# Attention taken two heads at a time, scores on halves of the array rows, values stationary, rows masked and exponentiated in place

## The chip, the cores and the metric

One Trainium2 chip, one of its cores. The metric is device time in microseconds (us) of one execution of the whole program, median of the runs shown.

## What is computed

Three stages follow one another. The first is attention in which each query keeps the keys of its 32 largest scores:

```python
# q, k, v: (2, 8, 576, 64)
scores = scale * np.matmul(q, k.transpose(0, 1, 3, 2))
kth = np.partition(scores, -top_k, axis=-1)[..., -top_k:-top_k + 1]
scores = np.where(scores >= kth, scores, -1000000000.0)
attn = np.exp(scores - np.max(scores, axis=-1, keepdims=True))
attn = attn / (np.sum(attn, axis=-1, keepdims=True) + 1e-09)
attn_out = np.matmul(attn, v)
```

The second takes the 1152 rows of 512 values, divides each by its root mean square, and passes it through a gated layer with 1536 hidden values: `silu(xn @ w_gate) * (xn @ w_val) @ w_out`. The third sends each row to one of 8 experts (the largest of 8 router logits), to at most 288 rows each, applies two matrices with a relu between them, and scales the row by its router probability.

## The kernel before

Rows are worked in nine tiles of 128. Tile 4 is the mixed one: its first 64 rows belong to batch 0 and its last 64 to batch 1, and the TensorE operations that depend on the batch are done for each half on 64 columns of the array (`halves`).

Attention and the gated layer run together in one list of steps, one head a step, 72 heads in all. In step n TensorE scores head n (`scores`, 128 rows of stationary queries, the other head's 64 rows of `q_cols` being zeros), ScalarE copies the scores into a ring of four rows `s_ring`, VectorE finds the 32nd largest in pairs of heads (MAX8 and MATCH_REPLACE8 in turn, then a last MAX8 that releases `th_set`), and ScalarE exponentiates into `p_ring` (L794). GpSimd turns the scores into ones and zeros by comparing with the threshold (L1120) and multiplies the exponentials by them (L1122). Four steps after the scores TensorE transposes the masked row in five blocks (`turn_probs`, L416), ScalarE copies them into `pt_ring`, and TensorE multiplies them as stationary operand with the values and a column of ones (`values`, L424, 65 columns). The ones give the sum of the row, and VectorE divides by it for a whole tile at a time (L966).

`due(n, offset)` says which tile's piece of the gated layer belongs to step n. A tile has six `ffn_block`s (gate and value columns 0 to 2, each twelve one-pass products of 512 columns: high part with high and low weights, L441 and L442, and low part with high weights, L445), 12 products for the output (`ffn_out`, L452), transposes of four blocks through the one bank `tb` (`turn`, L387; queries, normed rows, three of hidden values, output), router logits (L519), and the ranks. `use` numbers the turns of `tb`; each user waits on `t_free` for the one before.

In the first steps the two gated weights are scaled and split into a high and a low part, in twelve pieces. ScalarE writes the high part (L811); for six pieces it also scales the raw weights and GpSimd subtracts (L1113), for the six of `VEC_PIECES` VectorE does both in one operation (L912). The gated layer of the first tile waits for them.

After the last tile is dispatched the expert loop runs; the change leaves it as it is.

## Time and profile before

| | |
|---|---|
| median of 3 runs | 726.35 us (724.54 to 726.97) |
| profiled execution: its own time | 726.65 us |
| its span, first to last instruction | 724.9 us |
| mean granted TensorE clock | 0.956 of full speed |
| busy: TensorE / VectorE / ScalarE / GpSimd | 661.2 / 479.6 / 266.0 / 284.1 us |

Busy time is counted from the start of an instruction to its modelled end; matmuls are pipelined, so their shown durations overlap, and the distance between two starts is what one costs in a full queue. A granted clock of 1.00 is 2.4 GHz, 0.50 is 1.2 GHz. A number of instructions stands behind an x.

### The profile page before, as it was taken

The page shows a single profiled execution, that of the slowest core. Times are in us where ns is not written, and L with a number is a line of the kernel's source. Part 1 is how long each engine was busy: PE and PEld are TensorE (multiplying, and loading weights), DVE is VectorE, ACT ScalarE, POOL GpSimd, SP SyncE. Part 2 cuts the span into 40 slices and gives each one's busy share as a digit, 9 for nine tenths or more (in the row PEclk, how much of TensorE's full clock was granted, in tenths as well). Part 3 has the DMA queues.
Part 4 walks back from the last instruction along what each step waited for, and adds up shares of the span by engine and source line. Part 5 has one row for each costly group of instructions (what it writes and reads, how often), then busy time and mean ns, then how long its engine had stood idle before and what let it go on. Part 6 is the DMA issues. An engine that isn't in the chain of part 4 may idle for free.

```text
span 724.9 us, 10575 instructions
## 1 busy us (share of the span) xinstructions
PE 661.2 (91%) x3862; PEld 542.7 (75%) x3862; DVE 479.6 (66%) x1092; ACT 266.0 (37%) x473; POOL 284.1 (39%) x234
## 2 busy tenths in 40 slices
PE   5495689999999999999999999999985999999994
PEld 3374567688687578688688687785745999999994
DVE  3999979989989979989989999872211011111110
ACT  4385466355354354354354354432210011111110
POOL 2566765554645545546455564650000011111001
PEclk9878689999999999999999999999995999999998
DMA  9999000000000000000000000000067577876501
GB/s 186 364 382 291 0 16 0 1 16 1 7 23 1 16 16 1 16 16 1 15 16 1 16 2 1 15 1 16 0 247 236 195 247 262 270 251 232 185 16 35
DMA packets 52908, 65.43 MB, mean 90 GB/s; under 512 B 32058, under 2 KB 32058, under 8 KB 52860
## 3 DMA queue, kind: packets, MB, share of 16 engines
q1 hardware_dynamic: 51116, 60.05, 26.1%
q0 software_dynamic: 1744, 4.76, 1.8%
q8 instruction: 28, 0.46, 0.3%
q14 instruction: 20, 0.16, 0.1%
HBM read 52.89 MB, written 12.30 MB: 90 GB/s over the span
## 4 chain that ended last, share of the span: by engine, by line
PE 80%; DVE 13%; ACT 2%; DMA 1%; issue 1%; POOL 1%; SPq 0%; POOLq 0%; DVEq 0%; ACTq 0%
PE ps L452 13%; PE ps L595 10%; PE ps L609 10%; PE ps L424 8%; PE ps L400 8%; PE ps L441 6%; PE ps L445 6%; PE ps L442 6%; PE ps L416 5%; PE ps L387 3%; DVE w_top L1009 3%; DVE m L1004 3%; DVE w_parts L912 3%; DVE w_top L996 2%; DVE m L985 1%
## 5 line engine op out<-in xcount | busy, mean ns | idle before, releaser
L1120 POOL TENSOR_SCALAR s_ring<-s_ring,m 128x576 f32<-128x576 f32 x72 | 126.2, 1753 | 167.7 <-DVE m L1013 149.3
L1009 DVE MATCH_REPLACE8 w_top<-m,w_top 128x576 f32<-128x576 f32 x144 | 105.8, 743 | 0.0
L1122 POOL TENSOR_TENSOR p_ring<-p_ring,s_ring 128x576 f32<-128x576 f32 x72 | 102.3, 1420 | 6.0
L424 PEld LDWEIGHTS ps<-arena,pt_ring 128*128 128x128 f32 (+1 forms) x800 | 90.5, 186 | 16.8 <-issue 9.1
L1004 DVE MAX8 m<-w_top 128x8 f32<-128x576 f32 x144 | 101.6, 747 | 0.0
L424 PE MATMUL ps<-arena,pt_ring 128*128 128x65 f32 (+1 forms) x800 | 92.0, 267 | 4.1 <-ACT pt_ring L668 4.1
L452 PE MATMUL ps<-wo_space,hid 128*128 128x512 f32 x216 | 95.7, 593 | 0.0
L400 PE MATMUL ps<-arena,q_cols 128*128 128x288 f32 (+1 forms) x320 | 91.7, 442 | 2.1 <-ACT q_cols L668 1.4
L441 PE MATMUL ps<-w_parts,x_hi 128*128 128x512 f32 x216 | 92.2, 427 | 1.2 <-ACT x_hi L668 0.8
L442 PE MATMUL ps<-w_parts,x_hi 128*128 128x512 f32 x216 | 85.1, 394 | 0.0
L668 ACT ACTIVATE pt_ring<-ps 128x640 f32<-128x640 f32 x72 | 50.6, 703 | 81.0 <-PE ps L416 80.8
L595 PE MATMUL ps<-arena,w_loads 128*128 128x168 f32 x512 | 76.6, 312 | 0.6 <-ACT arena L668 0.6
L1129 POOL DMA_INDIRECT out_rows<-arena,s_ring x16 | 15.1, 942 | 157.9 <-DVE arena L1032 155.5
L609 PE MATMUL ps<-arena,w_loads 128*128 128x168 f32 x512 | 75.8, 307 | 0.6 <-issue 0.6
L595 PEld LDWEIGHTS ps<-arena,w_loads 128*128 128x128 f32 x512 | 75.5, 195 | 0.9 <-ACT arena L668 0.9
L416 PE MATMUL ps<-ident,p_ring 128*128 128x128 f32 x360 | 55.5, 288 | 20.4 <-POOL p_ring L1122 20.4
L609 PEld LDWEIGHTS ps<-arena,w_loads 128*128 128x128 f32 x512 | 73.2, 190 | 0.9 <-issue 0.9
L452 PEld LDWEIGHTS ps<-wo_space,hid 128*128 128x128 f32 x216 | 39.6, 190 | 43.0 <-issue 43.0
L400 PEld LDWEIGHTS ps<-arena,q_cols 128*128 128x128 f32 (+1 forms) x320 | 52.4, 195 | 14.3 <-issue 3.5
L416 PEld LDWEIGHTS ps<-ident,p_ring 128*128 128x128 f32 x360 | 43.4, 154 | 25.2 <-POOL p_ring L1122 23.0
L445 PE MATMUL ps<-w_parts,x_lo 128*128 128x512 f32 x216 | 59.3, 396 | 3.0 <-DVE x_lo L918 3.0
L985 DVE MAX8 m<-s_ring 128x8 f32<-128x576 f32 x72 | 52.0, 748 | 12.9 <-ACT s_ring L668 12.9
(116 smaller groups left out, 797.7 us busy)
## 6 DMA issues: line engine op xcount, KB each, us to landing
w_loads<-in_moe_w SPq DMA_DIRECT2D x16, 2048.0 KB, 9.0
dispatched_rows<-hid SPq DMA_DIRECT2D x18, 260.0 KB, 7.7
w_loads<-in_moe_w_gate SPq DMA_DIRECT2D x1, 3072.0 KB, 10.6
w_loads<-in_moe_w_val SPq DMA_DIRECT2D x1, 3072.0 KB, 18.1
wo_space<-in_moe_w_out SPq DMA_DIRECT2D x1, 3072.0 KB, 13.7
arena<-dispatched_rows SPq DMA_DIRECT2D x8, 341.2 KB
out_rows<-hid SPq DMA_DIRECT2D x9, 256.0 KB, 4.9
q_space<-in_q SPq DMA_DIRECT2D x8, 256.0 KB, 3.0
```

What stands on the lines that cost most here:

```text
L400: last = mm(ps[r0:r1, half, 0:HS], q_cols[:, h, r0:r1], kT[b][:, h // 2, half * HS:(half + 1) * HS], start=True, stop=True)
L416: last = tr(pt_ps[:, j * P:(j + 1) * P], p_ring[:, u % PR, j * P:(j + 1) * P], ident[:])
L424: last = mm(ao_ps(u % H, r0, r1), pt_ring[:, u % 2, j * P + r0:j * P + r1], vs[b][:, j, u % H, :], start=(j == 0), stop=(j == KC - 1))
L441: mm(bank, x_hi[:, c * P:(c + 1) * P], w_hi[:, c, :], start=(c == 0), stop=False)
L442: mm(bank, x_hi[:, c * P:(c + 1) * P], w_lo[:, c, :], start=False, stop=False)
L445: last = mm(bank, x_lo[:, c * P:(c + 1) * P], w_hi[:, c, :], start=False, stop=(c == CD - 1))
L452: last = mm(blk[0], hid[:, c * P:(c + 1) * P], wo_s[:, c, :], start=(c == 0), stop=(c == CF - 1))
L595: last = mm(ps[:, 2 + n % 2, (f % 2) * MAIN:(f % 2 + 1) * MAIN], w1_s[par][:, c, f * P:(f + 1) * P], xT[par][:, c, :], start=(c == 0), sto ...
L609: last = mm(ps[:, 4 + n, (d % 2) * MAIN:(d % 2 + 1) * MAIN], w2_s[par][:, f, d * P:(d + 1) * P], hT[:, f, :], start=(f == 0), stop=(f == C ...
L1004: vec.max(m8[:, u % 8, i, :], w_top[:, a, :]).then_inc(s["top_step"], 1)
L1009: vec.match_replace(w_top[:, a, :], m8[:, u % 8, i, :], w_top[:, a, :], NEG).then_inc(s["top_step"], 1)
L1120: gp.tensor_scalar(sc, sc, m8[:, n % 8, TOPK // 8 - 1, 7:8], None, ALU.is_ge).then_inc(s["pchain"], 1)
```

## The change

- Work goes in slots of two heads (36 of them, `g`), and what lies beside is placed in thirds of a slot: ALPHA, BETA, GAMMA. `due(n, at, k)` puts third k of tile t into slot 6 + 4t + k // 3. SLOTS is 44.
- The two heads of a slot are scored on the upper and the lower 64 rows of the array, into two pairs of banks, in turns (`scores`). `q_cols` holds no zeros; the copy of the queries applies the scale.
- The keys of the second head stand in another order, so that the rests of 64 keys of both heads lie side by side and one transpose turns them both: 9 transposes for two heads, not 10 (`turn_probs`, `turn_rest`).
- In `values` the values are stationary, 64 columns of the array a head, and the turned probabilities move, 128 columns; the output is the attention transposed, so a transpose back is added (XB), and the sums come from the exponential's accumulator (`den`).
- ScalarE computes `relu(FAR * (threshold - score))` (`marks`), GpSimd subtracts that from the row, and ScalarE exponentiates the row where it lies (`probs`). The comparison and the product on GpSimd and the two small operations a pair for the bias on VectorE are gone.
- GpSimd divides by the sums (power -1 and a product), multiplies gate and value, which ScalarE copies out first (`value_block`), and does the low part of all twelve pieces of the weights, for odd pieces with the scaling. Pieces go two a slot, in slots 2 to 7 (`pieces`).
- The output product comes in four parts of three (OUT). The column order of the output products is the same.

The diff, cut to its core (added and kept lines; what was there before is printed above):

```diff
+ALPHA, BETA, GAMMA = 0, 1, 2
+XB, XN = -3, -1
+G, V = (0, 2, 4), (1, 3, 5)
+HID = (3, 5, 7)
+OUT = (6, 7, 8, 9)
+X2, LOGITS, LEXP, RANK, SEND = 10, 11, 13, 14, 15
+LAST = 16
...
+        pt_ps, last_ps, oT_ps = ps[:, 4, :], ps[:, 0, HS:HS + P], ps[:, 1, HS:HS + P]
         blk = [ps[:, 5, :], ps[:, 6, :]]
         tb = ps[:, 7, :]
...
+        def due(n, at, k):
+            t, off = divmod(n - FIRST - k // 3, HP)
+            return t if k % 3 == at and off == 0 and 0 <= t < NT else None
...
+        def key_spans(a, half):
+            if a == 0:
+                return [(half * HS, half * HS + HS)]
+            return [(S - KL, S), (0, HS - KL)] if half == 0 else [(HS - KL, S - KL)]
...
+        def pieces(n, at):
+            m = 2 * (n - 2) + at
+            return (m,) if at < 2 and 0 <= m < 4 * FB else ()
...
+                if g % HP == 0:
+                    pe.wait_ge(s["q_copied"], g // HP + 1)
+                hp = g % HP
+                for half in range(2):
+                    for a, r0, r1, b in streams(g):
+                        at = 0
+                        for k0, k1 in key_spans(a, half):
+                            last = mm(ps[r0:r1, 2 * a + half, at:at + k1 - k0], q_cols[a * D:(a + 1) * D, hp, r0:r1],
+                                      kT[b][a * D:(a + 1) * D, hp, k0:k1], start=True, stop=True)
+                            at += k1 - k0
+                        if half == 1:
+                            last.then_inc(s["s_done"], 1)
...
+            def turn_probs(g, a):
+                pe.wait_ge(s["masked"], 2 * g + a + 1)
+                if g > 0 or a > 0:
+                    pe.wait_ge(s["pt_copied"], 3 * g + 1 if a else 3 * g - 1)
+                for j in range(KC - 1):
+                    last = tr(pt_ps[:, j * P:(j + 1) * P], s_ring[:, g % SR, a, a * KL + j * P:a * KL + (j + 1) * P], ident[:])
                 last.then_inc(s["pt_done"], 1)
+            def turn_rest(g):
+                pe.wait_ge(s["s_copied"], min(2 * (g + 2) + 1, 2 * NG))
+                tr(last_ps, s_ring[:, g % SR].rearrange("p a n -> p (a n)")[:, S - KL:S + KL], ident[:]).then_inc(s["pt_done"], 1)
+            def values(g):
+                pe.wait_ge(s["pt_copied"], 3 * g + 3)
+                hp = g % HP
+                spans = [(0, P, kind_of(g))] if kind_of(g) != "mix" else [(0, 64, 0), (64, P, 1)]
+                for r0, r1, b in spans:
                     for j in range(KC):
+                        for a in range(2):
+                            at = a * 512 + j * P if j < KC - 1 else 1024
+                            last = mm(oT_ps[a * D:(a + 1) * D, r0:r1], vs[b][:, j, 2 * hp + a, :],
+                                      pt[:, at + r0:at + r1], start=(j == 0), stop=(j == KC - 1))
+                            if r1 == P and j == KC - 1:
+                                last.then_inc(s["pv_done"], 1)
...
+                    pe.wait_ge(s["k1_copied"], KC)
+                dense_first = n + 1 >= HP
+                if dense_first:
+                    dense(n, ALPHA)
+                if n + 1 < NG:
+                    scores(n + 1)
+                if not dense_first:
+                    dense(n, ALPHA)
...
+                for i in (2 * n - 2, 2 * n - 1):
+                    if 0 <= i < KC:
+                        if i == 0:
+                            pe.wait_ge(s["k_in1"], 16 * KC)
+                            pe.wait_ge(s["k_acted"], KC - 1)
+                        if i >= 2:
+                            pe.wait_ge(s["k1_copied"], i - 1)
+                        turn_keys(1, i, blk[i % 2])
+                dense(n, BETA)
+                if probs:
+                    turn_probs(g, 1)
+                    turn_rest(g)
+                dense(n, GAMMA)
+                if probs:
                     if g == 0:
+                        pe.wait_ge(s["v_in0"], 16 * (KC + 1))
+                        pe.wait_ge(s["v_padded"], 2 * B)
+                    if g == MIX * HP:
+                        pe.wait_ge(s["v_in1"], 16 * (KC + 1))
+                    values(g)
             pe.wait_ge(s["seen_set"], NT)
             mm(tb[:, 0:E], ones[:], seen[:], start=True, stop=True).then_inc(s["t_full"], 1)
...
+            def value_block(tt, i):
+                act.wait_ge(s["blk_full"], tt * 6 + 2 * i + 2)
+                if i == 0:
+                    act.wait_ge(s["t_full"], use["xn", tt] + 1)
+                else:
+                    act.wait_ge(s["val_done"], tt * 3 + i)
+                nc.scalar.activation(xrow[:], blk[1], ACT.Copy, scale=rinv[:, 1:2]).then_inc(s["val_copied"], 1)
...
+            def split_weights(m):
+                raw, hi, _, half, cols = split_piece(m)
+                if m == 0:
+                    act.wait_ge(s["g_in"], 16)
+                    act.wait_ge(s["wg_in"], 16)
+                if m == 2:
+                    act.wait_ge(s["wv_in"], 16)
+                for c in half:
+                    nc.scalar.activation(hi[:, c, cols], raw[:, c, cols], ACT.Copy, scale=gain[:, c:c + 1]).then_inc(s["w_hi_set"], 1)
+                if m % 2 == 0:
+                    act.wait_ge(s["w_hi_set"], 2 * m + 2)
+                    for c in half:
+                        nc.scalar.activation(raw[:, c, cols], raw[:, c, cols], ACT.Copy, scale=gain[:, c:c + 1]).then_inc(s["w_scaled"], 1)
...
+            def marks(g, a):
+                act.wait_ge(s["far_set"], g + 1)
+                if g > 0:
+                    act.wait_ge(s["lowered"], 2 * g + a - 1)
+                nc.scalar.activation(z_pair[:, a, :], s_ring[:, g % SR, a, :], ACT.Relu, scale=-FAR,
+                                     bias=far[:, a:a + 1]).then_inc(s["marked"], 1)
+            def probs(g, a):
+                t, h = g // HP, 2 * (g % HP) + a
+                act.wait_ge(s["lowered"], 2 * g + a + 1)
+                act.wait_ge(s["bias_set"], g + 1)
+                if t >= 2:
+                    act.wait_ge(s["den_step"], 2 * t - 2)
+                row = s_ring[:, g % SR, a, :]
+                nc.scalar.activation(row, row, ACT.Exp, bias=nbias[:, 2 * (g % 2) + a:2 * (g % 2) + a + 1],
+                                     accum_out=den[:, t % 2, h:h + 1]).then_inc(s["masked"], 1)
+            def turned_probs(g, part):
+                act.wait_ge(s["pt_done"], 3 * g + part + 1)
+                if g > 0 and part == 0:
+                    act.wait_ge(s["pv_done"], 2 * g)
+                if part < 2:
+                    copy(pt[:, part * 512:(part + 1) * 512], pt_ps).then_inc(s["pt_copied"], 1)
+                else:
+                    copy(pt[:, 1024:PT], last_ps).then_inc(s["pt_copied"], 1)
+            def out_columns(g):
+                act.wait_ge(s["pv_done"], 2 * g + 2)
+                if g >= HP and g % HP == 0:
+                    act.wait_ge(s["t_full"], use["xb", g // HP - 1] + 1)
+                copy(oT[:, g % HP, :], oT_ps).then_inc(s["o_copied"], 1)
...
+                if here:
+                    marks(g, 0)
+                    marks(g, 1)
+                if 0 <= g - 1 < NG:
+                    out_columns(g - 1)
+                if here:
+                    probs(g, 0)
+                dense(n, ALPHA)
+                if n + 1 < NG:
+                    score_rows(n + 1, 0)
+                if n % HP == 2 and n // HP + 1 < NT:
+                    q_columns(n // HP + 1)
+                t = due(n, ALPHA, XB)
+                if t is not None:
+                    raw_rows(t)
+                if here:
+                    probs(g, 1)
+                if n + 1 < NG:
+                    score_rows(n + 1, 1)
+                if here:
+                    turned_probs(g, 0)
+                for i in (2 * n - 2, 2 * n - 1):
+                    if 0 <= i < KC:
+                        act.wait_ge(s["k_turned"], KC + i + 1)
+                        keys(1, i, blk[i % 2]).then_inc(s["k1_copied"], 1)
+                dense(n, BETA)
+                if here:
+                    turned_probs(g, 1)
+                    turned_probs(g, 2)
+                dense(n, GAMMA)
...
+                if n >= NG:
+                    beside(n - 1, GAMMA)
+                    beside(n, ALPHA)
+                    beside(n, BETA)
                     continue
+                done = n * 12
                 for a in range(2):
+                    dve.wait_ge(s["s_copied"], 2 * n + a + 1)
+                    if n >= 2:
+                        dve.wait_ge(s["bias_set"], n - 1)
+                    vec.max(m8[:, 2 * (n % 2) + a, 0, :], s_ring[:, n % SR, a, :]).then_inc(s["top_step"], 1)
                 for a in range(2):
...
+                    raw, hi, lo, half, cols = split_piece(m)
+                    pool.wait_ge(s["w_hi_set"], 2 * m + 2)
+                    if m % 2:
+                        for c in half:
+                            gp.tensor_scalar(raw[:, c, cols], raw[:, c, cols], gain[:, c:c + 1], None, ALU.mult).then_inc(s["pchain"], 1)
+                        pool.wait_ge(s["pchain"], 4 + m + 1)
+                    else:
+                        pool.wait_ge(s["w_scaled"], m + 2)
+                    gp.tensor_tensor(lo[:, half[0]:half[1] + 1, cols], raw[:, half[0]:half[1] + 1, cols],
+                                     hi[:, half[0]:half[1] + 1, cols], ALU.subtract).then_inc(s["w_lo_set"], 1)
+                t = due(n, at, XB)
+                if t is not None:
...
+                    pool.wait_ge(s["masked"], (t + 1) * H)
+                    gp.tensor_scalar(rden[:], den[:, t % 2, :], EPS_SUM, None, ALU.add).then_inc(s["den_step"], 1)
+                    pool.wait_ge(s["den_step"], 2 * t + 1)
+                    gp.tensor_tensor(rden[:], rden[:], nones[:], ALU.pow).then_inc(s["den_step"], 1)
+                    pool.wait_ge(s["den_step"], 2 * t + 2)
+                    pool.wait_ge(s["t_free"], use["xb", t] + 1)
+                    rows = xrow[:].rearrange("p (h d) -> p h d", h=H)
+                    gp.tensor_tensor(rows, rows, rden[:].rearrange("p (h a) -> p h a", a=1).broadcast_to([P, H, D]),
+                                     ALU.mult).then_inc(s["normed"], 1)
+                t = due(n, at, XN)
...
+                for i in range(FB):
+                    t = due(n, at, V[i])
+                    if t is not None:
+                        hb = hid[:, i * 512:(i + 1) * 512]
+                        pool.wait_ge(s["silu_done"], t * 3 + i + 1)
+                        pool.wait_ge(s["val_copied"], t * 3 + i + 1)
+                        gp.tensor_tensor(hb, xrow[:], hb, ALU.mult).then_inc(s["val_done"], 1)
+            for n in range(SLOTS):
+                g = n - 1
+                if 0 <= g < NG:
+                    pool.wait_ge(s["th_set"], 2 * g + 2)
+                    two = m8[:, 2 * (g % 2):2 * (g % 2) + 2]
+                    if g > 0:
+                        pool.wait_ge(s["marked"], 2 * g)
+                    gp.tensor_scalar(far.rearrange("p (a w) -> p a w", w=1), two[:, :, TOPK // 8 - 1, 7:8], FAR, None,
+                                     ALU.mult).then_inc(s["far_set"], 1)
+                    if g > 1:
+                        pool.wait_ge(s["masked"], 2 * g - 2)
+                    gp.tensor_scalar(nbias[:, 2 * (g % 2):2 * (g % 2) + 2].rearrange("p (a w) -> p a w", w=1), two[:, :, 0, 0:1], -1.0, None,
+                                     ALU.mult).then_inc(s["bias_set"], 1)
+                    for a in range(2):
+                        row = s_ring[:, g % SR, a, :]
+                        pool.wait_ge(s["marked"], 2 * g + a + 1)
+                        gp.tensor_tensor(row, row, z_pair[:, a, :], ALU.subtract).then_inc(s["lowered"], 1)
+                dense(n, ALPHA)
+                dense(n, BETA)
```

## Rows read from the trace of the kernel before

**Rows 1.** Busy time by stretch: two early ones, mixed tile's, a plain tile's.

```profile
core 0: us, PE busy (x) PEld busy (x) DVE busy (x) ACT busy (x) POOL busy (x), PEclk, DMA share, GB/s
...
75.00:90.00 15.00, 9.78 (x39) 8.37 (x40) 14.93 (x30) 7.38 (x12) 10.65 (x7) 0.61 0.00 1
...
185.30:238.90 53.60, 53.60 (x305) 39.76 (x305) 50.04 (x117) 24.15 (x44) 28.25 (x22) 1.00 0.04 11
238.90:293.20 54.30, 54.30 (x377) 39.58 (x377) 48.91 (x116) 24.33 (x44) 27.50 (x21) 1.00 0.04 11
345.00:396.80 51.80, 51.80 (x285) 40.65 (x284) 48.85 (x116) 23.99 (x44) 27.90 (x22) 1.00 0.04 11
```

**Rows 2.** The chain that ended last, in order of time: start, us, what.

```profile
133.30 3.44 PE ps L452 x8
...
372.96 0.97 PE ps L400 x4
...
494.61 3.49 PE ps L452 x8
...
527.33 3.44 PE ps L452 x8
```

**Rows 3.** Timeline of TensorE inside a plain tile: start, us, what.

```profile
376.57 1.22 PE L424 MATMUL ps<-arena,pt_ring 128*128 128x65 f32 x10
377.63 0.72 PE L416 MATMUL ps<-ident,p_ring 128*128 128x128 f32 x5
378.18 1.14 PE L400 MATMUL ps<-arena,q_cols 128*128 128x288 f32 x4
...
379.39 0.39 PE L442 MATMUL ps<-w_parts,x_hi 128*128 128x512 f32 x1
...
381.95 0.60 PE L387 MATMUL ps<-ident,hid 128*128 128x128 f32 x4
382.39 0.78 PE L424 MATMUL ps<-arena,pt_ring 128*128 128x65 f32 x6
```

**Rows 4.** Timeline of TensorE in the mixed tile: scores, then values.

```profile
218.41 0.72 PE L416 MATMUL ps<-ident,p_ring 128*128 128x128 f32 x5
219.05 1.20 PE L400 MATMUL ps<-arena,q_cols 128*64 128x288 f32 x8
...
220.52 0.39 PE L442 MATMUL ps<-w_parts,x_hi 128*128 128x512 f32 x1
...
256.20 1.20 PE L424 MATMUL ps<-arena,pt_ring 128*64 128x65 f32 x20
257.33 0.50 PE L441 MATMUL ps<-w_parts,x_hi 128*128 128x512 f32 x1
```

**Rows 5.** Groups by line and shape, whole span: busy us, mean ns, idle before.

```profile
L1120 POOL TENSOR_SCALAR s_ring<-s_ring,m 128x576 f32<-128x576 f32 x72 | 126.2, 1753 | 167.7 <-DVE m L1013 149.3 <-ACT p_ring L794 18.4
...
L1122 POOL TENSOR_TENSOR p_ring<-p_ring,s_ring 128x576 f32<-128x576 f32 x72 | 102.3, 1420 | 6.0
...
L794 ACT ACTIVATE p_ring<-s_ring,nbias 128x576 f32<-128x576 f32 x72 | 55.4, 770 | 0.2
...
L668 ACT ACTIVATE s_ring<-ps 128x576 f32<-128x576 f32 x72 | 46.9, 652 | 32.1 <-PE ps L400 25.2 <-POOL p_ring L1122 6.1
...
L901 DVE SCALAR_TENSOR_TENSOR hid<-ps,rinv,hid 128x512 f32<-128x512 f32 x27 | 20.1, 743 | 6.8 <-PE ps L445 6.8
...
L1113 POOL TENSOR_TENSOR w_parts<-w_loads,w_parts 128x1024 fp32r<-128x1024 f32 x6 | 16.1, 2686 | 0.0
...
L966 DVE TENSOR_TENSOR xrow<-ao,rden 128x512 f32<-128x512 f32 x9 | 11.4, 1263 | 0.3
...
L735 ACT ACTIVATION_READ_ACCUMULATOR hid<-xrow 128x1 f32 x9 | 1.8, 200 | 0.0
```

**Rows 6.** Timeline of the start, all engines: start, us, what.

```profile
1.83 0.94 POOL L1071 MEMSET q_cols<- 128x1024 f32 x1
...
32.18 1.41 DVE L1013 MAX8 m<-w_top 128x8 f32<-128x576 f32 x2
```

More of the change, by code:

```diff
@@ L9 @@
+import math
 from contextlib import ExitStack
@@ L57, in build @@
     HS = S // 2
-    VW = D + 1
     HP = H // 2
+    NG = NT * HP
     CAP = capacity
@@ L388, in turn @@
                 last.then_inc(s["t_full"], 1)
-            def scores(u):
-                t, h, kind = u // H, u % H, kind_of(u)
-                if u > 0:
-                    pe.wait_ge(s["s_copied"], u)
-                if h == 0:
-                    pe.wait_ge(s["t_free"], use["q", t] + 1)
-                for r0, r1, b in halves(kind):
-                    for half in range(2):
-                        last = mm(ps[r0:r1, half, 0:HS], q_cols[:, h, r0:r1],
-                                  kT[b][:, h // 2, half * HS:(half + 1) * HS], start=True, stop=True)
-                last.then_inc(s["s_done"], 1)
@@ L709, in dense @@
[L709 to L721 removed]
+                if t > 0:
+                    act.wait_ge(s["s_done"], scored(t * HP - 1))
@@ new lines, in dense @@
+            def dense(n, at):
+                for m in pieces(n, at):
+                    split_weights(m)
+                t = due(n, at, XN)
+                if t is not None:
+                    act.wait_ge(s["t_full"], use["xn", t] + 1)
+                    copy(x_hi, tb).then_inc(s["x_hi_set"], 1)
+                    act.wait_ge(s["normed"], t + 1)
+                    nc.scalar.activation(sqr, xrow[:], ACT.Square,
+                                         scale=float(DM) ** -0.5, accum_out=ssq[:, 0:1]).then_inc(s["x_sum"], 1)
+                for i in range(FB):
+                    t = due(n, at, G[i])
@@ L742, in dense @@
                     copy(dcol, tb).then_inc(s["t_free"], 1)
-                t = due(n, 11)
+                for i in range(FB):
+                    t = due(n, at, HID[i])
+                    if t is not None:
+                        act.wait_ge(s["t_full"], use[f"h{i}", t] + 1)
+                        copy(hid[:, i * 512:(i + 1) * 512], tb).then_inc(s["t_free"], 1)
+                t = due(n, at, LOGITS)
                 if t is not None:
@@ L1087, in _, with dense @@
             gp.memset(drow[:, DM:ROW], 0.0).then_inc(s["z_set"], 1)
-            for n in range(STEPS):
-                t = due(n, VEC_RANK)
+            def dense(n, at):
+                t = due(n, at, SEND)
                 if t is not None:
```

526 lines of the change are left out of this document (191 added, 335 removed).

## The prediction

> **What bounds the kernel now.** I read the busy times by stretch first, then the chain that ended last, then TensorE's own timeline, then the groups. In a plain tile TensorE is busy all of the 51.8 us at full clock, VectorE 48.85 of them, ScalarE and GpSimd about half [rows 1]. So between the first and the last output product TensorE is the bound, VectorE is close behind, and the other two have room. The start is another stage: from 75 to 90 us VectorE is busy 14.93 of 15 us, TensorE 9.8 at a granted clock of 0.61 [rows 1], because VectorE works on the weight pieces beside the search. The chain cuts the run into parts by the first part of the output product: it starts for tile 0 at 133.3, for tile 7 at 494.6, for tile 8 at 527.3 [rows 2]. I price the change in the three parts before, between and after these, and leave the experts' part alone.
>
> **One plain tile on TensorE.** Distances between starts give what an item costs. The five transposes of a head take 0.55 us, or 0.11 each; the scores and the block behind them 3.77, of which the scores are 0.97 [rows 2, 3], so a block is 2.8; a turn of four is 0.44 [rows 3]. Output products cost 0.43 an instruction (eight in 3.44), 10.3 a tile [rows 2]. The values of a head, ten instructions, are 1.06 [rows 3]. So attention is 5.15 for two heads (scores 1.94, transposes 1.1, values 2.12), 20.6 a tile, and 31.2 stay: output 10.3, six blocks about 17.1, six turns 2.6, and 1.2 for logits and ranks.
>
> After it, for two heads: nine transposes 0.99. For scores, two streams of 0.97 each, if the halves of the rows overlap, take 0.97 together, plus 0.1 for the short product of 64 keys; and the array changes its division twice. The mixed tile shows such a division, of columns: eight score instructions instead of four, and yet from the transposes before them to the second product behind them 2.11 us against 1.76 [rows 3, 4]. So halves of the columns do overlap, and the two changes cost 0.35 together. I take 1.4 for the scores. For values, ten pairs of instructions with 128 moving columns cost what a one-column-block transpose costs, 0.107, if a pair overlaps: 1.07; with 0.25 for the changes 1.32. (Twenty instructions of half width took 1.13 in the mixed tile [rows 4], so issuing them is no bound.) The sum is 3.7 instead of 5.15, four times a tile: -5.8. The transpose back adds 0.44. TensorE's work is then 46.5 us a tile.
>
> No row shows halves of the rows. The Trainium skill (TensorEngine Tiling (Array Packing), Key Properties) says that tiles operate independently, and that a change of tiling mode drains the engine; the second is the 0.35 above, the first would speak for overlap here as well. Without overlap the scores cost 2.4.
>
> **VectorE** loses three products by the value block, 0.74 each, and the division, 1.27 to 1.5 plus small ones [rows 5]: from 48.85 it falls to about 44.7. It is not the bound if nothing is late.
>
> **ScalarE** gains two marks of 0.77 and two accumulator reads of 0.2 for a slot, three copies of value blocks, one of raw rows, and four small ones of the output columns [rows 5]: from 24 to about 32 us a tile. **GpSimd** loses the comparison, 1.75 a head, keeps a two-operand pass of 1.42 [rows 5], and gets three products of 512 columns (1.27 each at that rate), about 21 us a tile instead of 28. Neither bounds a plain tile by its sum. Their order does in one place.
>
> **The fourth slot of a tile (n % 4 == 1).** It holds little dense work: the last output part 2.6, scores 1.4, turns XB, X2, XN 0.44 each, logits 0.8. I walked it from TensorE's start of it, in the order of the queues. The second head's transposes need the bank that ScalarE empties in `turned_probs(g, 0)`, and in ScalarE's queue there stand before it: output copy (ends 3.3), score copy (waits for scores, 4.0, ends 4.7), raw rows (5.2), exponential with accumulator (6.1), score copy (6.6), then the copy itself (7.1). TensorE is there at 5.3 and waits 1.9. Then XN turns (8.2), ScalarE makes the high part (9.1), VectorE the low part (9.8), and only this frees `tb` for the logits, behind which the values are queued: another 1.7. In the other three slots a block or an output part stands between, and I found no wait. So a tile costs 46.5 + 3.6 = 50.1, against 51.8. Behind the logits ScalarE's copy of them holds back the next marks, but these are needed only 5 us later.
>
> From tile 0 to tile 7, seven intervals, the kernel takes 361.3 us [rows 2]. After: 7 x 50.1 = 350.7, less 1.4 for the scores that the last of them lacks, plus about 3.5 for the mixed tile, which costs 4.3 now (53.6 + 54.3 - 2 x 51.8, [rows 1]): 352.8. **-8.5 us.**
>
> **The start.** Slots 0 and 1 go as now, the second pair's search ends at 33.5 [rows 6], without its bias operations near 32. In slots 2 to 7 GpSimd and ScalarE work by turns. From the release of the threshold: marks at 1.1, the two subtractions end at 2.6 and 4.0, the first exponential at 3.6; four ScalarE passes of an even piece, 0.67 apart (0.65 is shown for a copy of 576, [rows 5]), end at 6.3; GpSimd's subtraction at 8.9 (2.69 shown, some of it contention). ScalarE's other copies and exponential end at 8.8, the odd piece's high part at 10.1; then GpSimd multiplies twice and subtracts, and only then looks at the next threshold. The multiply of 512 is shown nowhere. Above lies the comparison, 1.75 for 576 or 1.55 for 512 [rows 5]; below a fill, 0.94 for 1024 or 0.47 for 512 [rows 6]. I take 1.2, near the two-operand pass (1.42 for 576), since it reads one operand less and compares nothing. That gives 15.1 a slot. Six slots are 91; second keys, queries, the first tile's division and root mean square, and two products by the value blocks add about 7; the last piece is done near 130. Behind it stand one block (2.8 at full clock), a turn and the values: tile 0's output starts near 135, not 133.3. **+1.7 us** (+6 with the comparison's price, -7 with the fill's). If TensorE's clock has fallen in the wait, the block costs up to 2.8 more.
>
> The Trainium skill (GPSIMD Engine Reference, Engine selection) calls one-input operations on GpSimd roughly line-rate. The comparison's row disagrees: it has one tensor input and takes 3.0 ns an element, more than the 2.5 of the two-operand pass. By that rule the lower end would hold, as in the third rival.
>
> **The end.** From tile 7's output to tile 8's now 32.7 us [rows 2], since the normed rows of tile 8 are ready beside it. After: slot 36 takes 10.5 (output 7.7, turn 0.4, transposes 1.0, values 1.3), slot 37 8.1 (output part 2.6, turn back 0.4, copy 0.8, GpSimd product 1.4, turn 0.4, high and low part 1.5, logits 0.9, each waiting for the last), slots 38 and 39 six blocks with turns and rank 18.0: 36.6. **+3.9 us.** The dispatch behind it keeps its chain.
>
> **Sum.** 726.65 (the profiled execution, 0.3 above the median) - 8.5 + 1.7 + 3.9 = 723.8 us. A measurement of this kernel can tell about 0.3%, 2.2 us, from no change.
>
> **Rivals.**
> 1. The row halves don't overlap (chance 0.10). For it: only column halves are shown. Scores cost 1.0 more a slot, 36 slots: 760, slower. It decides from 1.5 us for a slot's scores on: 0.08 above mine, over 36 slots, takes back the whole gain.
> 2. TensorE's clock falls in the waits of the fourth slot (0.08). For it: the two waits lie within one short slot, and from 75 to 90 us the clock was 0.61. Against it: there the engine was idle 5.2 of 15 us [rows 1], here it would be 3.6 of 50. I put half of the fourth slot's work at 1.2 GHz, about 3 us a tile: 749, slower.
> 3. GpSimd's multiply costs as the fill, and the start is VectorE's and ScalarE's (0.12): -9 us, 715.
> 4. The changes of division cost almost nothing, since they are between long streams (0.10): -0.59 a slot over 36 slots, 703.
> 5. GpSimd holds the start at the comparison's price and further waits of 0.5 us a tile come up in the longer hand-over between the three engines (0.10): 732.
>
> The forecast's own case has 0.50, with 714 to 735: a wait of 1 us a tile more or less is 7 us, the start 4 either way. The range that leaves out no more than 2 in 10 is 703 to 745. Chances: of the forecast's case a little over half lies below 724.5, with rivals 3 and 4 that is 0.47 faster; within 0.3% 0.17; slower 0.36.
>
> **What would show it.** A plain tile of about 50 us with TensorE idle 3 to 4 us of it, all in the fourth slot, ahead of `turn_probs(g, 1)` and of the logits; a slot's scores 1.4 and values 1.3 from start to start; VectorE near 45 a tile; slots 3 and 4 of the start about 15 us apart, GpSimd busy most of it; the first output part near 135 us. Wrong would be a score block of 2 us or more, VectorE or ScalarE without idle time in a plain tile, or a start paced by VectorE.

## The result: 2.7% slower

The changed kernel takes 745.98 us (median of 4 runs, 744.79 to 746.95), the kernel before beside it 726.66. The ratio is 1.0267, 95% interval 1.0234 to 1.0300. The forecast was 723.8, with a range up to 745.0: wrong in its sign, and the time lies 1 us outside.

The profiled execution has a span of 745.0 us. The busy times of the parts that answer to [rows 1]: an early stretch, the mixed tile's scores, a plain tile, and the end part.

```profile
core 0: us, PE busy (x) PEld busy (x) DVE busy (x) ACT busy (x) POOL busy (x), PEclk, DMA share, GB/s
75.00:90.00 15.00, 6.34 (x35) 4.63 (x31) 7.64 (x15) 9.70 (x19) 11.26 (x10) 0.61 0.01 2
191.80:245.30 53.50, 50.39 (x306) 36.15 (x303) 43.63 (x102) 31.69 (x68) 22.21 (x28) 0.94 0.04 11
...
349.30:402.90 53.60, 50.49 (x294) 36.46 (x292) 44.64 (x102) 31.48 (x68) 22.10 (x28) 0.94 0.04 11
506.70:548.00 41.30, 36.95 (x163) 25.88 (x162) 4.89 (x21) 12.89 (x29) 11.57 (x15) 0.92 0.02 7
```

VectorE, ScalarE and GpSimd have come to what was forecast (44.6, 31.5 and 22 us a tile). TensorE is idle some 3 us a tile, and the column PEclk, 1.00 in all three tiles of [rows 1], is 0.94 in both tiles here and 0.94 to 0.97 in the seven. The chain that ended last gives the parts, as [rows 2] did. Of the start:

```profile
126.12 6.02 issue
132.14 0.77 PE ps L480
...
137.40 1.24 PE ps L465 x20
138.64 2.77 PE ps L492 x6
```

The wait of 6.02 us has no releaser in the chain. GpSimd's own queue shows what ended then (at 132.04), the low part of the last weight piece:

```profile
129.69 2.35 POOL L1155 TENSOR_TENSOR w_parts<-w_loads,w_parts 128x1024 fp32r<-128x1024 f32 x1
```

The chain of the end part:

```profile
509.85 0.64 issue
...
510.72 0.66 PE ps L449 x4
...
526.34 1.85 PE ps L547 x8
528.18 0.63 PE ps L480
...
548.19 3.87 PE ps L492 x9
```

Tile 0's output part starts at 138.64 (133.30 before), tile 7's at 506.65, tile 8's at 548.19 (so 368.0 and 41.5 between them, 361.3 and 32.7 before), and 196.8 us follow (197.6). The 20.1 us are +5.3 at the start, +6.7 over seven tiles, +8.8 in the end part and -0.8 behind it.

TensorE's timeline in the fourth slot of a plain tile, and the first block behind it (start, us, what; in brackets the idle time before, and who ended it):

```profile
364.15 1.36 PE L437 MATMUL ps<-arena,q_cols 64*128 64x288 f32 x10
365.44 0.66 PE L420 MATMUL ps<-ident,oT 128*128 128x128 f32 x4
365.94 0.60 PE L449 MATMUL ps<-ident,s_ring 128*128 128x128 f32 x4
366.88 0.63 PE L420 MATMUL ps<-ident,drow 128*128 128x128 f32 x4 [0.34 <-ACT xrow L707]
368.66 0.63 PE L449 MATMUL ps<-ident,s_ring 128*128 128x128 f32 x4 [1.15 <-ACT pt L707]
369.12 0.27 PE L455 MATMUL ps<-ident,s_ring 128*128 128x128 f32 x1
369.23 0.60 PE L420 MATMUL ps<-ident,xrow 128*128 128x128 f32 x4
371.45 1.72 PE L547 MATMUL ps<-wr,hid 128*128 128x8 f32 x8 [1.62 <-DVE x_lo L992]
373.10 2.40 PE L465 MATMUL ps<-pt,arena 128*64 128x128 f32 x20
375.43 0.80 PE L480 MATMUL ps<-w_parts,x_hi 128*128 128x512 f32 x1
376.02 0.63 PE L481 MATMUL ps<-w_parts,x_hi 128*128 128x512 f32 x1
376.45 0.63 PE L480 MATMUL ps<-w_parts,x_hi 128*128 128x512 f32 x1
...
379.77 1.36 PE L437 MATMUL ps<-arena,q_cols 64*128 64x288 f32 x10
```

Both forecast waits are there, ahead of `turn_probs(g, 1)` at 368.66 and of the logits at 371.45, released by the engines that the walk through the queues had named. With the small one at 366.88 they are 0.5 + 1.34 + 1.78 = 3.6 us from start to start, as forecast. What was not in the sum comes right behind: the logits take 1.65 us (373.10 - 371.45), where they take 0.9 to 1.0 in the kernels below that keep the clock (0.8 was forecast); the values 2.33, where they are 1.24 at full clock; the block from 375.43 to 379.77 takes 4.34, where it is 2.8. Its first products follow each other at 0.43 us, not at 0.23: the clock is at 1.2 GHz instead of 2.4. In the end part the same: logits 1.84, and a block of 4.7 us from 528.18 on.

Groups of instructions that the change brings or alters on GpSimd (busy us, mean ns):

```profile
L1186 POOL TENSOR_TENSOR hid<-xrow,hid 128x512 f32<-128x512 f32 x27 | 34.8, 1289 | 105.9 <-ACT xrow L739 105.6
L1155 POOL TENSOR_TENSOR w_parts<-w_loads,w_parts 128x1024 fp32r<-128x1024 f32 x12 | 28.3, 2361 | 14.5 <-ACT w_loads L763 14.0
L1151 POOL TENSOR_SCALAR w_loads<-w_loads,gain 128x512 f32<-128x512 f32 x12 | 18.8, 1574 | 8.3 <-ACT w_parts L759 8.3
L1163 POOL TENSOR_TENSOR rden<-rden,nones 128x8 f32<-128x8 f32 x9 | 15.1, 1675 | 0.8
...
L1175 POOL TENSOR_TENSOR ssq<-ssq,nhalf 128x1 f32<-128x1 f32 x9 | 5.2, 582 | 0.7
```

The multiply of 512 (L1151) takes 1.57 us, the price of the comparison for its size [rows 5]; 1.2 had been taken. The Trainium skill (GPSIMD Engine Reference, Engine selection) calls one-input operations on GpSimd roughly line-rate. The trace doesn't bear that out: 1.57 us is 3.1 ns a column, and the product of two tensors of the same size (L1186) takes 1.29.

### The profile page after: what moved, and what is told of

Same layout as the page of the kernel before. It is cut to its first block, busy times and chain, and to the rows that moved or that the text cites. A ratio compares the mean times of both kernels' runs of the same rounds, so it can differ in the third digit from the quotient of the medians.

```text
span 745.0 us, 11068 instructions
## 1 busy us (share of the span) xinstructions
PE 636.8 (85%) x3942; PEld 502.3 (67%) x3942; DVE 420.5 (56%) x956; ACT 332.4 (45%) x698; POOL 263.4 (35%) x303
## 3 DMA queue, kind: packets, MB, share of 16 engines
q1 hardware_dynamic: 51148, 60.05, 25.4%
## 4 chain that ended last, share of the span: by engine, by line
PE 74%; ACT 10%; POOL 7%; issue 4%; DVE 3%; DMA 1%; SPq 0%; ACTq 0%; POOLq 0%; DVEq 0%
PE ps L492 12%; PE ps L634 10%; PE ps L648 10%; PE ps L480 7%; PE ps L481 7%; PE ps L484 6%; PE ps L465 6%; PE ps L437 5%; PE ps L449 4%; PE ps L420 3%; POOL w_loads L1151 2%; ACT s_ring L846 2%; PE ps L547 2%; POOL w_parts L1155 2%; ACT w_parts L759 2%
## 5 line engine op out<-in xcount | busy, mean ns | idle before, releaser
L1205 POOL TENSOR_TENSOR s_ring<-s_ring,z_pair 128x576 f32<-128x576 f32 x72 | 100.5, 1416 | 43.4 <-ACT z_pair L836 43.4
L480 PE MATMUL ps<-w_parts,x_hi 128*128 128x512 f32 x216 | 97.9, 453 | 6.0 <-issue 6.0
L481 PE MATMUL ps<-w_parts,x_hi 128*128 128x512 f32 x216 | 92.1, 426 | 0.0
L449 PE MATMUL ps<-ident,s_ring 128*128 128x128 f32 x288 | 47.6, 291 | 31.3 <-ACT pt L707 22.6
L1186 POOL TENSOR_TENSOR hid<-xrow,hid 128x512 f32<-128x512 f32 x27 | 34.8, 1289 | 105.9 <-ACT xrow L739 105.6
L437 PE MATMUL ps<-arena,q_cols 64*128 64x288 f32 (+5 forms) x400 | 54.0, 413 | 21.0 <-ACT oT L707 18.9
L1043 DVE MAX8 m<-s_ring 128x8 f32<-128x576 f32 x72 | 51.7, 748 | 34.6 <-ACT s_ring L707 34.6
L836 ACT ACTIVATE z_pair<-s_ring,nbias 128x576 f32<-128x576 f32 x72 | 51.9, 772 | 42.7 <-POOL nbias L1196 42.7
L449 PEld LDWEIGHTS ps<-ident,s_ring 128*128 128x128 f32 x288 | 34.9, 148 | 45.5 <-issue 30.2
L846 ACT ACTIVATE s_ring<-s_ring,nbias 128x576 f32<-128x576 f32 x72 | 55.5, 771 | 17.5 <-POOL s_ring L1205 17.5
L465 PE MATMUL ps<-pt,arena 128*64 128x128 f32 (+1 forms) x800 | 58.7, 305 | 4.7 <-ACT pt L707 4.7
L437 PEld LDWEIGHTS ps<-arena,q_cols 64*128 64x128 f32 (+1 forms) x400 | 35.6, 192 | 38.4 <-issue 38.0
```

The lines of the kernel that those rows point to most:

```text
L437: last = mm(ps[r0:r1, 2 * a + half, at:at + k1 - k0], q_cols[a * D:(a + 1) * D, hp, r0:r1], kT[b][a * D:(a + 1) * D, hp, k0:k1], start=Tru ...
L449: last = tr(pt_ps[:, j * P:(j + 1) * P], s_ring[:, g % SR, a, a * KL + j * P:a * KL + (j + 1) * P], ident[:])
L465: last = mm(oT_ps[a * D:(a + 1) * D, r0:r1], vs[b][:, j, 2 * hp + a, :], pt[:, at + r0:at + r1], start=(j == 0), stop=(j == KC - 1))
L480: mm(bank, x_hi[:, c * P:(c + 1) * P], w_hi[:, c, :], start=(c == 0), stop=False)
L481: mm(bank, x_hi[:, c * P:(c + 1) * P], w_lo[:, c, :], start=False, stop=False)
L1205: gp.tensor_tensor(row, row, z_pair[:, a, :], ALU.subtract).then_inc(s["lowered"], 1)
```

## The experiments

Times are medians of 4 runs, and of 10 for fill_both, fill_second_wait and odd_pieces_on_vector. Ratios are to the kernel before on the same chip, which took 726.7 us beside the change, 727.2 beside the three just named and logits_third_later, and 726.4 beside the others. "First part" is the start of tile 0's first output part, "tile" a seventh of the time from there to tile 7's, "end part" the time from tile 7's to tile 8's. These are read from TensorE's timelines, the granted clock in the middle from a stretch between 140 and 475 or 500 us.

| kernel | time us | ratio, 95% interval | first part | tile | end part | clock in the middle |
|---|---|---|---|---|---|---|
| the change | 745.98 | 1.0267 [1.0234, 1.0300] | 138.6 | 52.6 | 41.4 | 0.95 |
| fill_both | 727.76 | 1.0005 [0.9993, 1.0017] | 139.4 | 50.1 | 38.7 | 1.00 |
| fill_second_wait | 726.80 | 0.9996 [0.9982, 1.0009] | 139.0 | 50.1 | 38.7 | 1.00 |
| early_second_exp | 737.14 | 1.0150 [1.0119, 1.0181] | 140.0 | 51.2 | 41.3 | 0.96 |
| logits_third_later | 720.58 | 0.9915 [0.9898, 0.9931] | 138.3 | 49.2 | 38.0 | 1.00 |
| odd_pieces_on_vector | 728.22 | 1.0022 [1.0010, 1.0035] | 119.0 | 52.6 | 41.4 | 0.94 |
| logits_later_and_odd_pieces | 703.88 | 0.9692 [0.9652, 0.9731] | 120.5 | 49.3 | 39.6 | 1.00 |
| all_three | 698.82 | 0.9632 [0.9602, 0.9662] | 120.4 | 48.5 | 38.0 | 1.00 |
| all_three_again | 698.69 | 0.9608 [0.9569, 0.9646] | 121.1 | 48.5 | 39.6 | 1.00 |
| all_three_start_filled | 695.88 | 0.9579 [0.9544, 0.9614] | 118.7 | 48.5 | 38.0 | 1.00 |
| heads_one_after_another | 746.86 | 1.0282 [1.0235, 1.0328] | 138.1 | 52.5 | 41.5 | 0.96 |
| second_head_on_first_rows | 1046.12 | 1.4406 [1.4345, 1.4466] | 123.5 | 51.7 | 39.5 | 1.00 |

### Is it the waits, or the clock behind them?

Products whose result nobody reads are put into the waits. What ends a wait is not touched, so the items behind it start when they did, but TensorE works meanwhile.

```
+            def fill(t, k):
+                pe.wait_ge(s["val_copied"], 3 * t + 3)
+                for _ in range(k):
+                    mm(blk[1], wg_hi[:, 0, 0:P], wg_hi[:, 0, 0:512], start=True, stop=True)
...
                     pe.wait_ge(s["r_in"], 16)
+                    fill(t, 7)
                     pe.wait_ge(s["t_free"], use["lg", t])
...
                 dense(n, BETA)
+                if probs and n % HP == 1 and n >= 9:
+                    fill((n - 9) // HP, 5)
```

**fill_both** has all of it.

> The changed kernel with products on TensorE that nobody reads, into the bank of the value block, which is free there: five of 512 columns (0.23 us each at full clock) ahead of the second head's transposes in the fourth slot, seven ahead of the logits. They fit into the two waits, so the waits end when they did. Theory 1 (idle time in the fourth slot lowers TensorE's clock, and the slow values, logits and first block behind it cost 3.5 us a tile): a granted clock of 0.99 or more in plain tiles, values behind the logits 1.24 instead of 2.33 us, tile 50.1 instead of 52.8, total near 724. Theory 2 (the clock falls through what TensorE does there, row halves and short products, not through idling): clock stays 0.94 to 0.97, total 744 to 748. Theory 3 (clock kept, but another engine sets the tile): clock 1.00, tile 52 or more, total above 740.

**fill_second_wait** has only the seven products ahead of the logits.

> As the run before, with the seven products ahead of the logits alone. Theory 1: if the second wait (1.8 us) is what takes the clock down, total near 724 as with both; if both waits together do, in between, 728 to 738. Theory 2: 744 to 748.

Useless work makes the kernel 18 to 19 us faster. The plain tile of fill_second_wait, from output part to output part, then its fourth slot:

```profile
340.60:391.10 50.50, 49.00 (x302) 35.02 (x300) 43.63 (x102) 31.61 (x68) 22.22 (x28) 1.00 0.04 11
```

```profile
359.97 0.63 PE L449 MATMUL ps<-ident,s_ring 128*128 128x128 f32 x4 [1.16 <-ACT pt L714]
...
360.90 1.87 PE L504 MATMUL ps<-w_parts 128*128 128x512 f32 x7
362.67 1.06 PE L554 MATMUL ps<-wr,hid 128*128 128x8 f32 x8
363.66 1.31 PE L465 MATMUL ps<-pt,arena 128*64 128x128 f32 x20
```

The wait of 1.16 is untouched, the logits start 4.48 us behind the turn at 358.19, where it was 4.57 in the changed kernel, and the values are back at 1.2 us. The clock is 1.00 in the tile, and this plain tile takes 50.4 us from output part to output part, where the forecast had 50.1 with its waits in it. A seventh of the whole stretch is 50.15, where it was 52.58. So the fall of the clock costs 7 x 2.4 = 17 us in the middle and 2.7 in the end part, and filling the second wait alone is enough to stop it. The first wait need not be filled.

**early_second_exp** takes the first wait away and leaves the second: in the fourth slot ScalarE exponentiates the second head ahead of its other copies.

```
                     probs(g, 0)
+                if here and n % HP == 1:
+                    probs(g, 1)
                 dense(n, ALPHA)
...
-                if here:
+                if here and n % HP != 1:
                     probs(g, 1)
```

> In the fourth slot of each tile ScalarE exponentiates the second head before it takes the output part's copies, so the wait of 1.3 us ahead of the second head's transposes should fall under 0.5 us; the wait of 1.8 us ahead of the router's logits stays. Theory (the clock falls behind the wait of 1.8 us by itself): the tile keeps its half-clocked stretch and goes from 52.6 to about 51.3 us, the end of tile 7 from 506.7 to about 497, the time 736 to 739, granted clock of the middle still 0.93 to 0.97. Rival (it takes both waits together to bring the clock down): the clock of the middle is 1.00, the tile 48.8 to 49.3 us, the time 720 to 723. Second rival (the wait moves to what ScalarE now does later, the row to be sent and the score copies): 744 to 748.

```profile
365.07 0.63 PE L449 MATMUL ps<-ident,s_ring 128*128 128x128 f32 x4 [0.41 <-ACT pt L707]
...
367.86 1.03 PE L547 MATMUL ps<-wr,hid 128*128 128x8 f32 x8 [1.62 <-DVE x_lo L994]
```

```profile
346.50:397.70 51.20, 48.84 (x294) 34.80 (x292) 43.52 (x102) 31.60 (x68) 22.09 (x28) 0.97 0.04 11
```

As the theory said: 737.1 us, the tile 51.2, the clock still down. The first wait goes from 1.15 to 0.41 and the tile gives back 1.4 us. Behind the second wait, of 1.62 us, the clock still falls: it is 0.94 in the first of the seven tiles and 0.97 in each of the others. The rival, that it takes both waits at full length, falls. Whether the second would do it without the short waits just before it (0.34 and 0.41 us here) was not tried.

**logits_third_later** takes the second wait away by order: the logits come a third of a slot later, behind the values and a whole block.

```
-X2, LOGITS, LEXP, RANK, SEND = 10, 11, 13, 14, 15
+X2, LOGITS, LEXP, RANK, SEND = 10, 12, 13, 14, 15
...
         for n in range(SLOTS):
+            turned("lg", due(n, ALPHA, LOGITS))
...
-            turned("lg", due(n, GAMMA, LOGITS))
```

> The logits one third of a slot later, behind the first gate block of the next tile, so that nothing in the fourth slot waits for VectorE's low part. Theory 1: the wait of 1.8 us goes and with it most of the slow stretch: tile 48.5 to 50, total 710 to 725. Theory 2: only the wait goes, 1.7 us in eight tiles: about 732. Theory 3 (the wait moves to the block's last four products, which need the low part): 738 to 746.

```profile
405.50 0.63 PE L449 MATMUL ps<-ident,s_ring 128*128 128x128 f32 x4 [1.15 <-ACT pt L707]
...
406.99 1.31 PE L465 MATMUL ps<-pt,arena 128*64 128x128 f32 x20 [0.31 <-ACT pt L707]
...
411.13 0.95 PE L547 MATMUL ps<-wr,hid 128*128 128x8 f32 x8
```

```profile
336.60:386.20 49.60, 47.25 (x295) 33.90 (x293) 43.51 (x102) 31.32 (x68) 22.11 (x28) 1.00 0.04 12
```

720.6 us: 25 less than the changed kernel and 0.9% less than the kernel before. The tile loses 2.4 us of clock, and the logits wait for nothing. Of the 1.8 us of their wait only 0.9 is won: the values now wait 0.31 for a copy, and the next turn of queries 0.55 for the copy of the logits. One constant and the place of one line in the turns' order are the whole difference between a slower and a faster kernel.

### The start

**odd_pieces_on_vector** gives the low part of the six odd weight pieces to VectorE, in one operation a half, as the kernel before had it. GpSimd keeps the subtraction of the even ones.

```
+                for m in pieces(n, at):
+                    if m % 2:
+                        dve.wait_ge(s["w_hi_set"], 2 * m + 2)
+                        raw, hi, lo, half, cols = split_piece(m)
+                        for c in half:
+                            vec.scalar_tensor_tensor(out=lo[:, c, cols], in0=raw[:, c, cols], scalar=gain[:, c:c + 1],
+                                                     in1=hi[:, c, cols], op0=ALU.mult, op1=ALU.subtract).then_inc(s["w_lo_vec"], 1)
...
                     if m % 2:
-                        for c in half:
-                            gp.tensor_scalar(raw[:, c, cols], raw[:, c, cols], gain[:, c:c + 1], None, ALU.mult).then_inc(s["pchain"], 1)
-                        pool.wait_ge(s["pchain"], 4 + m + 1)
+                        continue
```

> The low part of the six odd pieces of the weights on VectorE, in one operation a half, as in the kernel before, all else as changed. Theory 1 (GpSimd paces the start, 15.3 us a slot in slots 2 to 7, 3.1 of it the two multiplies, 2.4 the subtraction): slots of 12.5 to 13.5, the first output part near 127 instead of 138.6, total near 735. Rival (ScalarE and VectorE are then as late, since the piece comes late in VectorE's slot and the two engines' two-input operations wait for each other): slots of 14.5 or more, total 741 to 746.

The stretch of 75 to 90 us:

```profile
75.00:90.00 15.00, 10.33 (x59) 7.78 (x58) 12.81 (x24) 10.06 (x22) 9.88 (x12) 0.74 0.00 1
```

728.2 us, and the first output part at 119.0, 19.6 us earlier: more than either account had it. VectorE is busy 12.8 of the 15 us, where it was 7.6. GpSimd's slots start 12.7 and 12.4 us apart (44.8, 57.5, 69.9), where they were 15.6 and 15.3 apart; 2.9 a slot is 17 us over six slots. The account had allowed VectorE's extra work to take much of this back; in fact its operations (909 ns a half) fell where it had been waiting. (The same operation averaged 1.60 us in the kernel before, L912; why it is shorter here was not looked into.) The tile and the end part are unchanged, so this edit and logits_third_later's should add.

**logits_later_and_odd_pieces** has both edits.

> Both edits that worked alone: logits a third of a slot later, and VectorE making the low parts of the odd weight pieces. By theory they act on different stretches and add: first output part at 119.0 us, seven tiles of 49.2, an end part of 38.0, 197 behind it, so a span of 698.4 and a time of about 700. Rival (the shorter start ends in a phase of the slots that brings other waits, as the end part's 41.4 may hide): 705 to 712.

703.9 us: start 120.5, tile 49.3, end part 39.6. By the medians the two gains add but for 1 us (25.4 + 17.8 against 42.1). Counted by the parts it is 3 us more than the sum: the start and the end part each came out 1.5 us longer, and both times it is the clock. Behind the same wait for tile 0's last low part it is 0.60 here and was 0.79 there (8.5 and 8 us up to the first output part).

```profile
112.00:120.50 8.50, 7.44 (x36) 5.80 (x36) 8.50 (x18) 1.87 (x4) 1.11 (x1) 0.60 0.00 0
```

```profile
111.00:119.00 8.00, 6.21 (x37) 4.91 (x37) 7.93 (x15) 2.45 (x6) 0.76 (x1) 0.79 0.00 0
```

The first line is of logits_later_and_odd_pieces, the second of odd_pieces_on_vector.

**all_three** has early_second_exp's edit as well, and **all_three_again** is the same kernel beside the next two.

> As the kernel with both edits, and the second head exponentiated earlier in the fourth slot. Theory: the wait of 1.15 us ahead of the second head's transposes goes as well, tile 48.1 us, time 7 x 1.1 below that kernel's: 692 when that one is at 700. Rival (ScalarE then copies the row to be sent and the scores later and TensorE waits there instead): within 2 us of that kernel, or slower.

> The kernel with the three edits once more, as the base for the two that follow: a ratio to the kernel before of 0.963, about 698 us.

```profile
316.70:365.50 48.80, 47.20 (x294) 33.84 (x292) 43.45 (x102) 31.32 (x68) 22.05 (x28) 1.00 0.04 12
460.70:500.30 39.60, 35.98 (x164) 24.95 (x163) 4.80 (x21) 12.93 (x29) 11.63 (x15) 0.96 0.02 7
```

698.8 and 698.7 us. The tile is 48.5, 0.75 below logits_later_and_odd_pieces; 1.1 was expected. TensorE's idle time in it is 1.6 us, in four waits of 0.3 to 0.55. The two profiles differ in the end part by 1.5 us, 38.0 against 39.6, where in the second the clock was down for a while (0.96) and in the first never (1.00), behind the same three waits of 0.8 us in a row that tile 8's normed rows need. So behind such a series of waits the clock falls in one profile and not in another.

**all_three_start_filled** puts four unread products into each of the two waits ahead of tile 0's last block.

```
                 dense(n, BETA)
+                if n == 7:
+                    fill(2, 4)
...
+                        if t == 0 and i == 2:
+                            fill(2, 4)
                         ffn_block(t, (wv_hi, wv_lo), i, blk[1])
```

> The kernel with the three edits, and four products that nobody reads in each of TensorE's two waits ahead of tile 0's last value block (1.75 and 2.04 us). Theory (those waits bring the clock down for the 3.4 us in which the block behind them runs): tile 0's first output part starts at 118.7 where it started at 120.4, all later parts as much earlier, 1.7 us below the base. Rival (the clock of the start is down for what TensorE did long before those waits, 0.50 to 0.58 from 60 to 90 us): within 0.5 us of the base, or slower by the part of the fills that sticks out of the waits.

```profile
90.00:118.70 28.70, 25.77 (x161) 19.62 (x159) 22.39 (x42) 21.82 (x42) 12.49 (x10) 1.00 0.04 10
```

The first output part starts at 118.7, 1.7 and 2.4 us earlier than in the two profiles of the base, at a clock of 1.00. In all_three_again the first of the two waits was 0.59 us and not 1.75, and the clock fell behind the second (2.04) all the same; the two fills were not tried one by one. The time, 695.9, is the lowest of all; its interval and the base's overlap (0.9544 to 0.9614, 0.9569 to 0.9646), so the gain is read from the traces and not proved by the times.

### What the halves of the rows are worth

**heads_one_after_another** issues the score products head by head.

```
-                for half in range(2):
-                    for a, r0, r1, b in streams(g):
+                for a, r0, r1, b in streams(g):
+                    for half in range(2):
```

> The changed kernel, with the nine score products of a slot issued head by head (both halves of the keys for the first head, then for the second) where they alternated between the halves of the array's rows. Theory (the block's 1.29 us for nine products come from two products on different row halves running at the same time, which needs them side by side in the queue): the block costs near twice that, 2.2 to 2.5 us, a tile about 4 us more, the time 770 to 785; the waits behind the blocks may take up to 1 us a slot of it back. Rival (the nine products are cheap for another reason, the shorter contraction of 64 rows): block 1.3 us, time 744 to 748.

The block is five products, which leave ten records; the "nine" above is a miscount. My theory of the order fell: the block still takes 1.29 us (393.34 - 392.05), the time is the same.

```profile
392.05 1.36 PE L437 MATMUL ps<-arena,q_cols 64*128 64x288 f32 x10
393.34 0.66 PE L449 MATMUL ps<-ident,s_ring 128*128 128x128 f32 x4
```

In the records of this run the second head's short product starts within 0.1 us of the first head's first, although two products of 288 columns stand ahead of it in the program; both kernels' records are in the same order. This left two accounts: overlap whatever the order, or products on 64 rows that are cheap in themselves.

**second_head_on_first_rows**, built on all_three, parts them: the second head's products read the first head's queries and keys, so all five stand on one half. It does not compute the second head's scores.

```
-                            last = mm(ps[r0:r1, 2 * a + half, at:at + k1 - k0], q_cols[a * D:(a + 1) * D, hp, r0:r1],
-                                      kT[b][a * D:(a + 1) * D, hp, k0:k1], start=True, stop=True)
+                            last = mm(ps[r0:r1, 2 * a + half, at:at + k1 - k0], q_cols[0:D, hp, r0:r1],
+                                      kT[b][0:D, hp, k0:k1], start=True, stop=True)
```

> The kernel with the three edits, but both heads' score products read the first head's queries and keys, so that all five products of a slot stand on the same 64 rows of the array: the second head's scores are not computed. Everything else, the instruction counts, columns and waits, is as it was. Theory (two products on different row halves run at the same time, whichever order they are issued in): the block goes from 1.3 to the 1.94 us of twice a head's 0.97 before, 0.65 a slot over 36 slots is 23 us, of which the waits ahead of the second head's transposes may give back up to 0.3 a slot: 710 to 722 us. Rival (products with a contraction of 64 rows are cheaper by themselves): within 2 us of the base, about 698.

```profile
373.18 2.32 PE L437 MATMUL ps<-arena,q_cols 64*128 64x288 f32 x10
375.43 0.65 PE L449 MATMUL ps<-ident,s_ring 128*128 128x128 f32 x4
```

The block takes 2.25 us instead of 1.29, the tile 51.7 instead of 48.5 (waits gave back 0.7 of the 3.8). So it is overlap: two halves of the rows run at once, worth 0.96 us a slot. That is the price of one head's scores before (0.97), so the second head's stream is hidden whole; the block costs some 0.3 us beyond its streams on two halves (1.29) and on one (2.25), which the expected 1.94 left out. This agrees with the Trainium skill (TensorEngine Tiling (Array Packing), Key Properties), by which tiles work in parallel. The whole time says nothing here: the other attention output sends the rows to other experts, and a part for overfull experts, skipped otherwise, runs for some 320 us more at the end.

## Why the prediction was wrong, point by point

- **TensorE's work and the waits of a tile: right.** Scores 1.29 (1.4 taken), values 1.24 (1.32), the waits 3.6 (3.6), a plain tile 50.4 once the clock is kept (50.1), all seven 351.0 (352.8). The 3.5 us put down for the mixed tile did not appear: the two intervals that hold it take 50.3 and 50.4 in fill_second_wait. Rival 1 is out, since the halves overlap. Rival 4 is out too, though beside their streams scores and values hold 0.4 us a slot and not the 0.6 taken.
- **The step that failed: the stalls of the fourth slot were put into the sum at their own length, with the work behind them at full clock.** The clock's fall stood beside it as rival 2, with 0.08. Its mechanism is what happened, and its size was nearly right (about 3 us a tile; measured 2.4, and 2.7 in the end part). Its chance was what was wrong. What misjudged the chance was the comparison of shares: "idle 5.2 of 15 us" against "3.6 of 50". A mean over a tile says nothing of this. What the runs show to count is where the idle time lies: with a wait of 1.6 us between a turn of 0.4 and logits of 0.9 the clock fell in each of the seven tiles, even with the first wait cut to 0.41; with the first wait at 1.15 us and without the second it fell in none. 19 of the 22 us between forecast and result are this, shown by fill_second_wait (726.8 us).
- **The start: +5.3 where +1.7 was forecast.** The last low part was ready at 132.1, "near 130" was said. The multiply was mis-sized (1.57, not 1.2), partly made up by a shorter subtraction (2.36, not 2.69), so the slots named in the forecast came out 15.6 and 15.3 us apart (15.1); two later slots were longer, 19.4 and 17.7, and the reciprocal of eight columns, 1.68 us, was not priced by itself. The rest, 2 us, is the block behind that wait of 6.0 us, which ran at the lower clock: 4.8 us instead of 2.8. That sentence stood in the prediction as a condition, and was left out of the sum. Rival 3 is out.
- **The end part: +8.8 where +3.9 was forecast.** At full clock it is 38.7, 2.1 more than the 36.6 counted: 1.2 of it is the wait ahead of the first head's transposes at 510.72, since the marks and the subtraction of that pair come behind the product of hidden values (L1186) on GpSimd. The other 0.9 was not traced. The clock adds 2.7.
- **The room on VectorE** was seen (44.7 a tile) but not in the start, where 7.4 of 15 us lay idle while GpSimd set the pace. That alone was worth 19.6 us.

## What to carry to other kernels

When work is taken from the engine that is the bound, look for the slot in which so little is left that its waits come out, and price what follows the wait at the lower clock as a case of its own: here 3.6 us of waits a tile cost another 2.4. Judge a wait by the work directly around it, not by the idle share of a tile. Before a rewrite is given up, try moving one short dependent item a third of a slot (25 us here), and look at which engine waits while a slower one sets the pace (18 us): the same change is worth -3.8% or +2.7%, depending on these edits.

## What the runs showed of the hardware

- Score products on the two halves of the rows run at the same time even when the program issues them head by head: 1.29 us in either order, 2.25 on one half.
- GpSimd's power takes 1.68 us for eight columns and 0.58 for one (L1163 and L1175 of the changed kernel). If the cost is linear between them, an estimate from two sizes, it is 0.16 us a column above 0.4. A multiply by a value per row takes 1.57 us for 512 columns, a product of two tensors 1.29 (L1186).
- Behind a wait of 1.6 us between short items, with shorter waits just before it, the clock fell to 1.2 GHz in every tile. With seven unread products in that wait it stayed at 2.4 GHz (fill_second_wait, granted clock 1.00).
